# Linear attention, routed experts and an MLP on one core: array forms grouped, routing moved behind the masks, counts read in one load

## Chip, cores and metric

One core of a Trainium2 chip runs the whole program in one launch. The metric is the device time in microseconds (us) of that core; lower is better. Engines are TensorE (PE), VectorE (DVE), ScalarE (ACT), GpSimd (POOL) and SyncE (SP), each with its own instruction queue; they order one another by semaphores.

## What is computed

Three stages follow one another on 2 x 768 = 1536 tokens of width 384 (8 heads of 48):

```python
for t in range(S):                      # per batch and head, 48 x 48 state
    y[t] = r[t] @ (state + (u * k[t]) outer v[t])
    state = w[:, None] * state + k[t] outer v[t]
logits = x @ w_gate                     # 8 experts; x is y with its heads side by side
local = sigmoid(x @ w_local)
e[s] = argmax(logits[s]) if s == 0 or local[s] < 0.5 else e[s - 1]
out[s] = softmax(logits[s])[e] * relu(x[s] @ w1[e]) @ w2[e]
result = out + relu(layernorm(out) * g_ln @ w_ch1) @ w_ch2
```

## The kernel before

**Attention.** The 1536 tokens are 12 chunks of 128 (NT = 12), the two batches (B = 2) in turn. Inside a chunk the recurrence is a masked product. The loop of each engine runs over i from 0 to 13 and works on three chunks at once: the scores of chunk i, output and state of chunk j = i - 1, and the routing logits of chunk i - 2. PE's order in iteration i is written by hand: scores of chunk i (L1128, 8 products whose operands fill 64 rows and 128 columns of the array), the three transposes of chunk i - 2's rows X (L1135, 128 x 128), then the turned output of chunk j in bank 0: for each of 4 head pairs two products of the state (L1149, 64 rows x 48 columns) and two of the masked scores (L1152, 128 rows x 48 columns), which add to the same columns; then logits of chunk i - 2 (L1165, 128 x 128), addition to the state (L1176, 128 rows x 64 columns), and the four transposes that turn the output back (L1183, 128 x 128). Every fp32 product is two passes in the trace, every transpose one. So L1149 and L1152 show 16 passes each, in groups of four.

DVE in iteration i: stores X of chunk i - 2 (L836, adds the bonus term dv), masks the scores of chunk i (L846, two instructions), adds the state (stsum, L853), scales the next chunk's keys (kT, L825), then the bonus's diagonal (L863, L865). ACT copies the transposed X (L620) for the logits, the turned output (L629), the logits (L632), and multiplies v by the diagonal in 8 small instructions (L609), four before and four behind the copy L629. POOL multiplies rT, rk, ks and the state. SP starts the loads of a chunk: tin 512 KB, kr 384 KB, v 192 KB. ACT starts the first two experts' weights in halves of 1536 KB, in iterations 2, 4, 6 and 8 (HALF_WEIGHTS).

**Routing.** It comes in two phases: chunks 0 to 7 during iterations 10 to 12 and chunks 8 to 11 behind the loop. A phase is, on DVE, choose (argmax and codes, L762 to L771), carry_on (a scan over the tokens, L777 to L782), chosen (one-hot and gate value, L789 to L800) and places (row numbers, L808 to L819), with small products on PE between them. Then POOL scatters each chunk's rows to HBM, sorted by expert (L518, 8 and 4 indirect DMAs). SP fills the tail of an expert's rows with zeros and loads the first 256 rows (xrow, L433). Behind places of the second phase DVE computes counts and writes them to meta, of which each engine loads its registers one by one (expert_regs, L305).

**Experts.** Tiles of 256 rows, here eight, one for each expert. Each fp32 weight is split into two parts, high (split_hi, L359, ACT) and low (split_lo, L364, POOL and DVE), in six pieces of 1024 columns; pieces 0 to 2 are w1, 3 to 5 w2. A product is three passes (L1203, L1204, L1205). Expert 0's pieces 0 and 1 are made low by POOL in iterations 10 and 11, pieces 2 to 5 by DVE in iterations 9, 11, 12 and 13 (LATE_LO). When all are done, SP loads expert 2's weights (two halves) over expert 0's raw ones. Then comes the MLP, in three groups of four chunks, and POOL scatters its rows to the output (L599).

## Time and profile before

| | before |
|---|---|
| median of 3 runs | 424.46 us (423.89 to 425.12) |
| the profiled execution's own time | 423.79 us |
| its span, first to last instruction | 422.2 us |
| PE busy | 384.4 us (91%) |
| DVE / ACT / POOL busy | 217.3 / 146.5 / 137.5 us |
| chain that ended last | PE 81%, DVE 7%, DMA 4%, POOL 3% |

The span is 1.6 us short of the time. Busy shares are means over stages that differ; the chain that ended last follows back, from the last instruction, what released each step. A row of the timeline gives start, length, engine, line, operation and, in brackets, how long the engine was idle before it and who ended that.

### The profile page before, as it was taken

How to read it: one execution, taken by the hardware profiler on the slowest of the kernel's cores; microseconds unless marked ns; L12 is line 12 of the kernel's file. 1: busy time of each engine (PE TensorE's matmuls, PEld its weight loads, DVE VectorE, ACT ScalarE, POOL GpSimd, SP SyncE). 2: the span in 40 equal slices, each digit the busy share in tenths (PEclk: the TensorE clock that was granted, in tenths of full speed). 3: DMA queues.
4: the chain of work that ended last, by engine and by line, in shares of the span. 5: the costliest groups of instructions: out<-in, count | busy, mean ns of one | idle time of the engine just before them, and what ended most of it. 6: DMA issues, size and time to landing. Idle time of an engine off the chain costs nothing.

```text
span 422.2 us, 7567 instructions
## 1 busy us (share of the span) xinstructions
PE 384.4 (91%) x2768; PEld 342.1 (81%) x2768; DVE 217.3 (51%) x412; ACT 146.5 (35%) x295; POOL 137.5 (33%) x134
## 2 busy tenths in 40 slices
PE   6799999872089999999999998999999999999993
PEld 6566766531079999999999998889998899988993
DVE  5776568856127466374664779585213552133110
ACT  0354566630035537255382553542002320022000
POOL 5986775745122605325053240400110001100010
PEclk9899999965579999999999999999999999999998
DMA  6999881019646957749556150600100001100001
GB/s 202 347 334 363 314 289 46 2 58 335 219 143 170 351 197 262 270 163 385 190 195 258 30 241 0 191 0 2 37 20 19 1 2 37 39 0 2 19 20 37
DMA packets 17018, 61.07 MB, mean 145 GB/s; under 512 B 2128, under 2 KB 9808, under 8 KB 14672
## 3 DMA queue, kind: packets, MB, share of 16 engines
q1 hardware_dynamic: 12240, 25.87, 18.1%
q10 hardware_dynamic: 2304, 26.74, 17.5%
q0 software_dynamic: 2432, 7.92, 4.9%
q8 instruction: 24, 0.39, 0.4%
q14 instruction: 18, 0.15, 0.1%
HBM read 49.42 MB, written 11.10 MB: 143 GB/s over the span
## 4 chain that ended last, share of the span: by engine, by line
PE 81%; DVE 7%; DMA 4%; POOL 3%; issue 3%; ACT 1%; SPq 0%; DVEq 0%; ACTq 0%; POOLq 0%
PE bank L1203 21%; PE bank L1205 21%; PE bank L1204 21%; PE bank L1152 3%; PE bank L1149 3%; POOL xsort L518 3%; PE bank L1128 2%; DMA tin<-in_rkT 2%; PE bank L1198 1%; PE bank L1165 1%; PE bank L1183 1%; PE bank L1135 1%; DMA xsort<-X,cpos 1%; PE bank L1176 1%; DVE split L364 1%
## 5 line engine op out<-in xcount | busy, mean ns | idle before, releaser
L359 ACT CAST split<-raw 128x1024 fp32r<-128x1024 f32 (+1 forms) x60 | 59.2, 1004 | 0.0
L1203 PE MATMUL bank<-xT,split 128*128 128x256 f32 x192 | 55.2, 287 | 2.1 <-DVE xT L910 2.1
L1205 PE MATMUL bank<-xT,split 128*128 128x256 f32 x192 | 55.0, 286 | 0.0
L1204 PE MATMUL bank<-xT,split 128*128 128x256 f32 x192 | 55.0, 286 | 0.0
L599 POOL DMA_INDIRECT out<-orow,cpos x12 | 11.6, 970 | 132.7 <-DVE orow L1039 132.7
L364 DVE TENSOR_TENSOR split<-raw,split 128x1024 fp32r<-128x1024 f32 (+1 forms) x40 | 51.1, 1292 | 1.9 <-ACT split L359 1.7
L1203 PE MATMUL bank<-split,h2T 128*128 128x384 f32 x144 | 48.7, 338 | 0.0
L1205 PE MATMUL bank<-split,h2T 128*128 128x384 f32 x144 | 48.2, 335 | 0.0
L1204 PE MATMUL bank<-split,h2T 128*128 128x384 f32 x144 | 48.2, 335 | 0.0
L364 POOL TENSOR_TENSOR split<-raw,split 128x1024 fp32r<-128x1024 f32 (+1 forms) x20 | 45.7, 2302 | 6.3 <-ACT split L359 6.2
L718 ACT ACTIVATE h2T<-bank 128x512 fp32r<-128x512 f32 x36 | 21.5, 598 | 72.9 <-PE bank L1205 71.7
L1051 DVE SCALAR_TENSOR_TENSOR h2T<-bank,h2T 128x512 fp32r<-128x512 f32 x36 | 24.9, 691 | 37.5 <-ACT h2T L718 37.4
L1203 PE MATMUL bank<-split,hT 128*128 128x384 f32 x128 | 43.7, 341 | 0.0
L1203 PE MATMUL bank<-split 128*128 128x512 f32 x108 | 42.1, 390 | 1.2 <-DVE split L942 1.2
L1205 PE MATMUL bank<-split,hT 128*128 128x384 f32 x128 | 42.8, 335 | 0.0
L1204 PE MATMUL bank<-split,hT 128*128 128x384 f32 x128 | 42.8, 334 | 0.0
L676 ACT ACTIVATE hT<-bank 128x512 fp32r<-128x512 f32 x32 | 19.1, 597 | 67.3 <-PE bank L1205 67.3
L1205 PE MATMUL bank<-split 128*128 128x512 f32 x108 | 42.1, 390 | 0.0
L1204 PE MATMUL bank<-split 128*128 128x512 f32 x108 | 42.1, 390 | 0.0
L958 DVE SCALAR_TENSOR_TENSOR hT<-bank,hT 128x512 fp32r<-128x512 f32 x32 | 22.0, 687 | 36.5 <-ACT hT L676 36.5
L1203 PEld LDWEIGHTS bank<-xT,split 128*128 128x128 f32 x192 | 37.6, 196 | 2.5 <-DVE xT L910 2.5
L1204 PEld LDWEIGHTS bank<-xT,split 128*128 128x128 f32 x192 | 37.6, 196 | 0.0
(161 smaller groups left out, 704.5 us busy)
## 6 DMA issues: line engine op xcount, KB each, us to landing
raw<-in_wexp ACTq DMA_DIRECT2D x14, 1536.0 KB, 8.3
tin<-in_rkT SPq DMA_DIRECT2D x12, 512.0 KB, 6.5
kr<-in_rows_kr SPq DMA_DIRECT2D x12, 384.0 KB, 5.7
raw<-in_wch ACTq DMA_DIRECT2D x2, 2304.0 KB, 9.4
xsort<-zeros SPq DMA_DIRECT2D x8, 388.0 KB, 5.7
X<-xsort SPq DMA_DIRECT2D x8, 388.0 KB, 5.8
ysort<-yrow POOLq DMA_DIRECT2D x8, 388.0 KB, 7.2
raw<-in_wexp SPq DMA_DIRECT2D x2, 1536.0 KB, 10.0
```

The source lines that it names most:

```text
L359: act.copy(hi, src).then_inc(s_hi, 1)
L364: eng.tensor_tensor(lo, src, hi.bitcast(F32), ALU.subtract).then_inc(s_lop if c < POOL_CK else s_lod, 1)
L518: pool.indirect_dma_start(out=xsort, out_offset=bass.IndirectOffsetOnAxis(ap=cpos[:, j:j + 1], axis=0), in_=X[:, j, :], in_offset=None).th ...
L676: act.activation(hT[:, 0, x * FU:(x + 1) * FU, :], bank[HB[x]][:].rearrange("p (f t) -> p f t", f=FU), ACT.Relu).then_inc(m_h, 1)
L718: act.activation(h2T[:, f, 0, :], bank[HB2[f % 3]][:], ACT.Relu).then_inc(f_ra, 1)
L958: dve.scalar_tensor_tensor(out=hT[:, 1, q, :].rearrange("p f t -> p (f t)"), in0=bank[HB[x]][:], scalar=0.0, in1=hT[:, 0, q, :].rearrange( ...
L1051: dve.scalar_tensor_tensor(out=h2T[:, f, 1, :], in0=bank[HB2[f % 3]][:], scalar=0.0, in1=h2T[:, f, 0, :].bitcast(F32), op0=ALU.max, op1=AL ...
L1149: pe.matmul(bank[0][halves[h], n * P:(n + 1) * P], state[b][h * HALF:(h + 1) * HALF, n, :], rT[j % 3][h * HALF:(h + 1) * HALF, n, :], star ...
L1152: last = pe.matmul(bank[0][halves[h], n * P:(n + 1) * P], vn[j % VRING][:, 2 * n + h, :], sc[b][:, h, n, :], start=False, stop=True)
L1203: pe.matmul(dst, stationary[0], moving[0], start=first, stop=False)
L1204: pe.matmul(dst, stationary[0], moving[1], start=False, stop=False)
L1205: return pe.matmul(dst, stationary[1], moving[0], start=False, stop=last)
```

## The change

The diff stands with one line of context; a line "..." leaves unchanged lines out. On PE, the eight products of L1149 come first, then the eight of L1152, then the addition to the state, the transposes of X, those of the output, and the logits last; the waits for v and for the masked scores move between the two groups. On ACT the eight bonus products come first and the copy of the transposed X behind that of the output. On DVE the next keys are scaled ahead of stsum, choose(0) comes behind the masks, places(0) ahead of them, and of expert 0's low parts only piece 2 is made in the loop; pieces 3 to 5 are made in the first expert tile. SP loads w1 of expert 2 as soon as expert 0's w1 is split, ACT its w2 in the first tile. meta is laid out so that one load reads ten counts, without checks of their bounds.

```diff
@@ -119,10 +119,10 @@
-M_TILES, M_BEFORE, M_ROWS, M_ENDS, M_GROUP = (i * E for i in range(5))
-M_BEHIND = M_GROUP + NG
-M_MORE = M_BEHIND + 1
-meta = sb("meta", [1, M_MORE + 1], I32)
+M_TILES, M_MORE, M_BEHIND, M_GROUP = 0, E, E + 1, E + 2
+M_ROWS, M_ENDS = 2 * E, 3 * E
+assert M_GROUP + NG <= M_ROWS
+meta = sb("meta", [1, M_ENDS + E], I32)
@@ -297,25 +297,29 @@
 HALF_WEIGHTS = (2, 4, 6, 8)
-LATE_LO = (NT - 3, NT - 1, NT, NT + 1)
 def need(eng, s, n):
...
+def load_many(eng, a, b, most):
+    return nc.values_load_multi_w_load_instructions(
+        meta[0:1, a:b], engines=(eng.engine,), min_val=0, max_val=most,
+        skip_runtime_bounds_check_because="counts of rows that there are, and of their tiles")[1]
+
 def expert_regs(eng, offsets=False):
...
     eng.wait_ge(s_meta, 1)
-    tiles = [eng.value_load(meta[0:1, M_TILES + e:M_TILES + e + 1], min_val=1, max_val=NT) for e in range(E)]
+    said = load_many(eng, M_TILES, M_BEHIND + 1, NT + E)
+    tiles = [nc.s_assert_within(said[e], 1, NT, skip_runtime_bounds_check_because="counts rounded up to tiles, "
+                                "at least one") for e in range(E)]
+    more = nc.s_assert_within(said[M_MORE], 0, NT, skip_runtime_bounds_check_because="one less than a number of tiles")
     before = [0]
...
         before.append(eng.snap(before[e] + tiles[e], min_val=0, max_val=NT + E))
-    rows = [eng.value_load(meta[0:1, M_ROWS + e:M_ROWS + e + 1], min_val=0, max_val=TOK)
-            for e in range(E)] if offsets else None
-    behind = eng.value_load(meta[0:1, M_BEHIND:M_BEHIND + 1], min_val=0, max_val=NT + E)
-    more = eng.value_load(meta[0:1, M_MORE:M_MORE + 1], min_val=0, max_val=NT)
-    return tiles, before, rows, behind, more
+    rows = load_many(eng, M_ROWS, M_ROWS + E, TOK) if offsets else None
+    return tiles, before, rows, said[M_BEHIND], more
@@ -362,6 +366,13 @@
     eng.tensor_tensor(lo, src, hi.bitcast(F32), ALU.subtract).then_inc(s_lop if c < POOL_CK else s_lod, 1)
+
+def first_w1_split(eng):
+    eng.wait_ge(s_lop, POOL_CK)
+    eng.wait_ge(s_lod, CK // 2 - POOL_CK)
+
+def first_w2_split(eng):
+    eng.wait_ge(s_lod, CK - POOL_CK)
@@ -414,8 +425,8 @@
             sp.dma_start(gcol[:], gain_in).then_inc(s_small, 16)
-    split_done(sp, 0)
-    load_weights(sp, 2)
+    first_w1_split(sp)
+    load_weights(sp, 2, (0,))
@@ -431,8 +442,6 @@
     sp.dma_start(xrow[:], xsort[0:MT, 0:D].rearrange("(h p) d -> p h d", p=P)).then_inc(m_first, 16)
-    sp.wait_ge(s_meta, 1)
-
     sp.sem_inc(m_in, 16)
@@ -443,18 +452,17 @@
+    tiles, before, _, _, _ = expert_regs(sp)
     for e in range(E):
-        tiles = sp.value_load(meta[0:1, M_TILES + e:M_TILES + e + 1], min_val=1, max_val=NT)
-        before = sp.value_load(meta[0:1, M_BEFORE + e:M_BEFORE + e + 1], min_val=0, max_val=NT + E)
-        with sp.Fori(0, tiles) as i:
-            load_rows(before + i, nc.s_assert_within(
+        with sp.Fori(0, tiles[e]) as i:
+            load_rows(before[e] + i, nc.s_assert_within(
                 i * MT + e * CAP, e * CAP, e * CAP + TOK,
...
             sp.wait_ge(s_fill, 16 * (e + 2))
-    groups = [sp.value_load(meta[0:1, M_GROUP + g:M_GROUP + g + 1], min_val=1, max_val=NT + E)
-              for g in range(NG)]
+    groups = [nc.s_assert_within(x, 1, NT + E, skip_runtime_bounds_check_because="a group's rows are of one expert at least")
+              for x in load_many(sp, M_GROUP, M_GROUP + NG, NT + E)]
     for g in range(NG):
@@ -603,9 +611,9 @@
 def _(act):
-    def dg_times_v(j, heads):
+    def dg_times_v(j):
         b = j % B
-        for h in heads:
+        for h in range(H):
             last = act.activation(dv[b][:, h, :], vn[j % VRING][:, h, :], ACT.Copy, scale=dg[b][:, h:h + 1])
@@ -615,23 +623,20 @@
             load_weights(act, half // 2, (half % 2,))
-        if i >= 2:
-            act.wait_ge(s_xt, i - 1)
-            act.copy(xTa[:], bank[7][:, 0:D]).then_inc(s_xc, 1)
         j = i - 1
...
             need(act, s_x, j - B + 1)
-            dg_times_v(j, range(H // 2))
+            dg_times_v(j).then_inc(s_dvp, 1)
             act.wait_ge(s_yp, j + 1)
...
         if i >= 2:
+            act.wait_ge(s_xt, i - 1)
+            act.copy(xTa[:], bank[7][:, 0:D]).then_inc(s_xc, 1)
             act.wait_ge(s_lp, i - 1)
             act.copy(LG[:, i - 2, :], bank[7][:, D:D + E + 1]).then_inc(s_lg, 1)
-        if 0 <= j < NT:
-            dg_times_v(j, range(H // 2, H)).then_inc(s_dvp, 1)
         if NT - CK <= i < NT:
@@ -685,6 +690,9 @@
                 relus(range(NU))
+                if starts and e == 0:
+                    first_w2_split(act)
+                    load_weights(act, 2, (1,))
@@ -835,9 +843,9 @@
                               bank[4][:].rearrange("p (h d) -> p h d", h=H)[:, :, 0:Dh], dv[j % B][:], ALU.add).then_inc(s_x, 1)
-        if i == ROUTED[0]:
-            dve.wait_ge(s_late, 1)
-            choose(0)
+        if i == ROUTED[0] + 2:
+            places(0)
+            split_lo(dve, 0, POOL_CK)
         if i < NT:
@@ -845,15 +853,16 @@
                                   causal[:].unsqueeze(1).broadcast_to([P, NP, P]), ALU.mult).then_inc(s_sc, 1)
-        if i == ROUTED[0] + 2:
-            places(0)
+        if i + 1 < NT:
+            scale_k(i + 1)
         if 0 <= j < NT - B:
...
                               ALU.add).then_inc(s_ss, 1)
-        if i + 1 < NT:
-            scale_k(i + 1)
+        if i == ROUTED[0]:
+            dve.wait_ge(s_late, 1)
+            choose(0)
         if i < NT:
@@ -867,9 +876,6 @@
             chosen(0)
-        if i in LATE_LO:
-            split_lo(dve, 0, POOL_CK + LATE_LO.index(i))
-    assert len(LATE_LO) == CK - POOL_CK
@@ -886,8 +892,7 @@
     dve.tensor_scalar(meta[:, M_MORE:M_MORE + 1], cnt[:, 4, E - 1:E], 1.0, None, ALU.subtract)
-    dve.tensor_copy(meta[:, M_ROWS:M_ROWS + E], cnt[:, 0, :])
-    link(dve.tensor_tensor(meta[:, M_BEFORE:M_BEFORE + E], cnt[:, 5, :], cnt[:, 4, :], ALU.subtract))
+    link(dve.tensor_copy(meta[:, M_ROWS:M_ROWS + E], cnt[:, 0, :]))
     for g in range(NG):
@@ -948,6 +953,8 @@
     xT_lo()
+    for c in range(CK // 2, CK):
+        split_lo(dve, 0, c)
     for e in range(E):
@@ -1128,43 +1135,23 @@
             last.then_inc(s_scp, 1)
-        if i >= 2:
-            pe.wait_ge(s_x, i - 1)
-            need(pe, s_lg, i - 2)
-            for q in range(KD):
-                last = pe.transpose(bank[7][:, q * P:(q + 1) * P], X[:, i - 2, q * P:(q + 1) * P], ident[:])
-            last.then_inc(s_xt, 1)
-        if i == ROUTED[0] + 2:
-            counts(0)
         j = i - 1
...
-            pe.wait_ge(s_v[j % VRING], 16 * (j // VRING + 1))
-            pe.wait_ge(s_sc, 2 * (j + 1))
             need(pe, s_st, j - B + 1)
...
                     pe.matmul(bank[0][halves[h], n * P:(n + 1) * P], state[b][h * HALF:(h + 1) * HALF, n, :],
-                              rT[j % 3][h * HALF:(h + 1) * HALF, n, :], start=True, stop=False)
+                              rT[j % 3][h * HALF:(h + 1) * HALF, n, :], start=(n == 0), stop=False)
+            pe.wait_ge(s_v[j % VRING], 16 * (j // VRING + 1))
+            pe.wait_ge(s_sc, 2 * (j + 1))
+            for n in range(NP):
                 for h in range(2):
                     last = pe.matmul(bank[0][halves[h], n * P:(n + 1) * P], vn[j % VRING][:, 2 * n + h, :], sc[b][:, h, n, :],
-                                     start=False, stop=True)
+                                     start=False, stop=(n == NP - 1))
             last.then_inc(s_yp, 1)
-        if i == ROUTED[0]:
-            pe.wait_ge(s_late, 1)
-            code_rows(0)
-        if i == ROUTED[0] + 1:
-            expert_columns(0)
-        if i >= 2:
-            pe.wait_ge(s_xc, i - 1)
-            if i == 2:
-                pe.wait_ge(s_small, 16 * 2)
-            for q in range(KD):
-                last = pe.matmul(bank[7][:, D:D + E + 1], xTa[:, q * P:(q + 1) * P], wg[:, q, :],
-                                 start=(q == 0), stop=(q == KD - 1))
-            last.then_inc(s_lp, 1)
         if 0 <= j < NT - B:
@@ -1176,12 +1163,33 @@
             last.then_inc(s_u, 1)
+        if i == ROUTED[0] + 2:
+            counts(0)
+        if i >= 2:
+            pe.wait_ge(s_x, i - 1)
+            need(pe, s_lg, i - 2)
+            for q in range(KD):
+                last = pe.transpose(bank[7][:, q * P:(q + 1) * P], X[:, i - 2, q * P:(q + 1) * P], ident[:])
+            last.then_inc(s_xt, 1)
+        if i == ROUTED[0]:
+            pe.wait_ge(s_late, 1)
+            code_rows(0)
+        if i == ROUTED[0] + 1:
+            expert_columns(0)
         if 0 <= j < NT:
...
             last.then_inc(s_bk, 1)
+        if i >= 2:
+            pe.wait_ge(s_xc, i - 1)
+            if i == 2:
+                pe.wait_ge(s_small, 16 * 2)
+            for q in range(KD):
+                last = pe.matmul(bank[7][:, D:D + E + 1], xTa[:, q * P:(q + 1) * P], wg[:, q, :],
+                                 start=(q == 0), stop=(q == KD - 1))
+            last.then_inc(s_lp, 1)
@@ -1248,6 +1256,8 @@
             pe.wait_ge(m_y, n + XR)
+            if e == 0:
+                first_w2_split(pe)
             second(n, 0, range(KF // 2))
@@ -1268,7 +1278,10 @@
-        split_done(pe, e)
+        if e == 0:
+            first_w1_split(pe)
+        else:
+            split_done(pe, e)
         if e < E - 1:
```

## Rows read from the trace of the kernel before

**Rows 1.** Stretches: length; PE, PEld, DVE, ACT, POOL busy; clock, DMA share, GB/s.
```profile
19.30:44.00 24.70, 24.70 (x305) 16.88 (x304) 16.91 (x28) 11.72 (x44) 19.60 (x35) 1.00 0.94 340
84.70:91.50 6.80, 5.68 (x37) 2.71 (x37) 3.77 (x10) 1.38 (x5) 2.33 (x2) 0.50 0.00 0
118.80:122.20 3.40, 3.40 (x16) 3.40 (x17) 0.00 (x0) 0.00 (x0) 0.00 (x0) 0.50 0.17 26
122.30:263.00 140.70, 140.06 (x999) 139.37 (x998) 86.66 (x128) 71.57 (x100) 47.94 (x30) 1.00 0.57 208
```

**Rows 2.** Chain that ended last, iteration 4 and an expert tile: start, length, what.
```profile
38.43 1.09 PE bank L1128 x16
...
40.00 0.35 PE bank L1149 x4
...
42.83 0.77 PE bank L1165 x6
43.60 0.60 PE bank L1176 x16
44.20 0.59 PE bank L1183 x4
...
146.77 0.66 PE bank L1198 x6
```

**Rows 3.** Timeline of all engines, iteration 4: start, length, engine, line, operation.
```profile
39.45 0.55 PE L1135 MATMUL bank<-ident,X 128*128 128x128 f32 x3
39.57 1.29 DVE L846 TENSOR_TENSOR sc<-bank,causal 128x512 f32<-128x512 f32 x2 [0.54 <-PE bank L1128]
...
40.04 0.48 ACT L620 COPY xTa<-bank 128x384 f32<-128x384 f32 x1 [1.69 <-PE bank L1135]
...
40.78 0.34 DVE L853 TENSOR_TENSOR stsum<-state,bank 128x192 f32<-128x192 f32 x1
...
41.04 0.69 DVE L825 TENSOR_TENSOR kT<-tin,wn 128x512 f32<-128x512 f32 x1
```

**Rows 4.** Timeline of DVE around the routing, iterations 10 to 13.
```profile
70.73 0.21 DVE L762 TENSOR_REDUCE mx<-LG 128x8 f32<-128x64 f32 x1
...
72.04 1.28 DVE L846 TENSOR_TENSOR sc<-bank,causal 128x512 f32<-128x512 f32 x2
...
81.89 0.17 DVE L789 COPY ec<-bank 128x8 f32<-128x8 f32 x1 [1.14 <-PE bank L1095]
...
84.08 1.22 DVE L364 TENSOR_TENSOR split<-raw,split 128x1024 fp32r<-128x1024 f32 x1
...
86.87 0.18 DVE L808 COPY tot<-region 128x8 f32<-128x8 f32 x1 [1.10 <-PE bank L1105]
...
93.58 0.56 DVE L836 TENSOR_TENSOR X<-bank,dv 128x384 f32<-128x384 f32 x1 [3.68 <-ACT dv L609]
```

**Rows 5.** Chain that ended last, from the scatter to the expert products.
```profile
88.87 2.08 POOL xsort L518
...
103.19 0.96 POOL xsort L518
...
106.98 5.12 DMA xsort<-X,cpos
...
112.17 2.88 DMA xrow<-xsort
...
118.72 0.58 PE bank L1203
```

**Rows 6.** DMA issues: queue, operation, count, KB each, median us from issue to landing.
```profile
raw<-in_wexp ACTq DMA_DIRECT2D x14, 1536.0 KB, 8.3
...
out<-orow,cpos POOLq DMA_INDIRECT x12, 2.6
```

**Rows 7.** Timeline of DVE in the first expert tile.
```profile
123.34 0.69 DVE L958 SCALAR_TENSOR_TENSOR hT<-bank,hT 128x512 fp32r<-128x512 f32 x1 [4.68 <-ACT hT L676]
```

**Rows 8.** Timeline of PE, iteration 12.
```profile
85.82 0.90 PE L1135 MATMUL bank<-ident,X 128*128 128x128 f32 x3 [2.71 <-DVE X L836]
```


## The prediction

> **What bounds the kernel now.** I read the busy time by stretch first. PE has no idle time in the attention loop (24.70 of 24.70 us, clock 1.00, which is 2.4 GHz), and none to speak of once the expert products run (140.06 of 140.70 us) [rows 1]. What lies between is the routing. So only two things can shorten this kernel: less PE time in the loop's iterations, and an earlier first expert product, at 118.72 us [rows 5]. What follows that product isn't touched and should come through unchanged, 303.5 us of the 422.2 us span.
>
> The chain through iteration 4 shows what an iteration is made of: 1.09 for the scores, 0.48 for the transposes of X (40.00 - 38.43 - 1.09), eight groups of four passes at 0.35 to 0.36 (together 42.83 - 40.00 = 2.83), 0.77 logits, 0.60 state, 0.59 transposes back: 6.36 us [rows 2]. Six transposes that run between products of the same form take 0.66 us, 0.11 each; three of them cost 0.48 and four 0.59 where the form changes before and behind them, so a change costs 0.14 to 0.15 us [rows 2]. A group of four passes is two pairs (the two heads of a pair run together) at 0.107 each, and 0.14 for the change: 0.355.
>
> **The change, part by part.**
>
> *Grouping the products.* L1149 and L1152 alternate eight times, which is eight changes; grouped there are two. Six go: 6 x 0.14 = 0.84 us per iteration. Each group becomes 8 x 0.107 + 0.14 + 0.01 = 1.01 us. Behind L1152 comes L1176, also 128 rows by half the columns, so that change may go too (0.14), and the two kinds of transposes and the logits are all 128 x 128: two more at 0.15. PE alone would need 6.36 - 0.84 - 0.44 = 5.1 us. It can't have it, for two waits that the old order covered.
>
> First wait, at L1176. It needs stsum of the same iteration, and stsum now stands behind kT. The scores start at 39.45 - 1.09 = 38.36; the masks start 1.21 later [rows 3]. Masks 1.21 (39.57 to 40.78), kT 0.69 less the 0.08 by which a follower overlaps it, stsum 0.34, hand-over 0.05: DVE is ready at 1.21 + 1.21 + 0.61 + 0.34 + 0.05 = 3.42 us. PE is there at 1.09 + 1.01 + 1.01 - 0.14 = 2.97 to 3.05. It waits some 0.4 us.
>
> Second wait, at the logits. Transposes of X start at 3.42 + 0.60 = 4.02. From their start to the end of ACT's copy took 40.04 + 0.48 - 39.45 = 1.07, and 0.05 to hand over [rows 3]: 5.14 us. Transposes back are done by 4.85, so PE waits 0.3 us. The logits take 0.77 [rows 2], and the iteration ends at 5.91 us.
>
> So an iteration shrinks by 0.45 us, not by 1.28. Iteration 1 has no such waits yet, and I take 0.7 there; iterations 2 to 9 are eight: 0.7 + 8 x 0.45 = 4.3 us at the start of iteration 10, which was at 38.36 + 5 x 6.36 = 70.16.
>
> *Bonus first on ACT.* ACT is busy 11.72 us in 24.70, which is 3.0 us of each 6.36 [rows 1]; of those, its copy of X alone is 0.48 [rows 3], so the eight products are at most 2.5. They now come in one piece at the start of an iteration, from iteration 6 on behind a high part of the weights (1 us). That ends at 3.5 at the latest; the turned output is made at 3.1, and its copy is wanted only by 4.35, behind the transposes of X. I cost it at nothing; if the copy came later still, each tenth would be a tenth in the six iterations from 6 on.
>
> *Routing of the first phase.* From iteration 10 on DVE sets the pace. Its work in sequence: masks at 1.21; from there to the end of the diagonal of iteration 11 it had 81.89 - 1.14 - 72.04 = 8.71 us without a wait; choose takes 72.04 - 70.73 = 1.31 and now lies inside; chosen 84.08 - 81.89 = 2.19; storing X 0.48; places and the hand-over 88.87 - 86.87 = 2.00 [rows 4, 5]. Sum: 15.9 us from the start of iteration 10 to the first scatter, against 18.7 before. What went are the split at 84.08 (1.14) and the waits of 1.14 and 1.10 us; choose, which lay beside PE's scores, gives 0.6 back.
>
> *Second phase and scatter.* Behind places comes one split (1.14), then X of chunk 11 at 16.8. From there to the second phase's scatter it took 103.19 - 93.58 = 9.61 us [rows 4, 5], and that work is the same: 26.4. But POOL needs 2.38 + 7 x 1.26 = 11.2 us for the eight indirect DMAs of the first phase (1.26 from the three steps between 103.19 and 106.98), so it is free at 27.1: POOL, not DVE, is late next. The last of four is issued at 27.1 + 3.8 = 30.9. It took 5.12 to land [rows 5], while the zeros moved, and both halves of expert 2's weights had started only behind DVE's last split (93.58 + 0.48 + 1.14, about 95.2); the output's scatters land in 2.6 [rows 6]. Now half of those weights start about 10 us before it, and the other half much later. Between the two I take the middle, 3.9: 34.8. From landing to the first expert product it is 118.72 - 112.10 = 6.62 [rows 5]: 41.4 us, against 118.72 - 70.16 = 48.6. That is 7.1 us.
>
> *Counts in one load.* No register load is on the chain; what released PE was xrow, landed at 112.17 + 2.88 [rows 5]. The counts are made behind places of the second phase, which moves forward by 4.3 + (103.19 - 70.16) - 26.4 = 10.9 us, and xrow by 4.3 + 7.1 = 11.4. The old loads would have lost half a microsecond of their cover, and cost at most that. One load costs nothing, and I book no gain. On SP and POOL the fewer loads lie beside PE's first tile.
>
> *Three low parts in the first tile.* DVE waits 4.68 us there before its first relu part [rows 7]; three splits at 1.14 take 3.4. Free. ACT starts expert 2's w2 behind its last relu of the tile, and reads it behind the first relu of the next. Between them PE has the 48 passes of w2 and 18 of w1, at the mean of 140.70 / 999 = 0.14 us [rows 1] 9.3 us; such a load lands in 8.3 [rows 6]. Free, with a microsecond to spare; beyond it ACT's high parts for expert 2 would be late, which PE reads a tile later. SP's start of w1, now before the zeros, is a queue entry more in front of them and one fewer behind.
>
> *Clock.* PE idles through the second phase and begins the expert products at 0.50 of its clock, for the 3.4 us of one row; the other cold row lasted 6.8 [rows 1]. Half clock costs at most half of its time, so a start as long as the other would cost 3.4 x 0.5 = 1.7 us more, and one as short nothing. It is nearest to the row at its own place; I take 0.3.
>
> **Sum.** 4.3 + 7.1 - 0.3 = 11.1 us. The profiled execution took 423.79 us (span 422.2 and 1.6 around it); it becomes 412.7. The median of the runs is 0.7 above that execution: 413.4 us.
>
> **Rivals.**
>
> *Grouping brings nothing (0.12).* If the 0.14 us belonged to each head pair and not to the change of form, both groups take 4 x 0.355 = 1.42 us. L1176 then starts at 3.93 with no wait for stsum, and the logits at 3.93 + 0.60 + 1.12 = 5.65; the iteration lasts 6.42. The loop loses 0.5 instead of winning 4.3, the routing keeps its 7.1: 423.8 - 6.3, or 418.2 us as a median. Against it: no gap stands between transposes and products of one form [rows 2]. The Trainium skill would land there too by another way (TensorEngine Tiling, Gotcha 1: PSUM Pressure): different row tiles cannot use one PSUM bank at the same time, and the two heads of L1149 lie in different rows and write bank 0. By that a grouped L1149 would take its 16 passes in turn, 1.7 us or more. The trace disagrees: four such passes and the change fit into 0.35 us, where four in turn at 0.107 would be 0.43 alone.
>
> *Neither wait holds (0.10).* If DVE and ACT keep up, PE's 5.1 us isn't reached either, since two iterations move 2 x 1088 + 1536 KB = 3.8 MB, at 340 GB/s [rows 1] 11.2 us: 5.6 each. Then 8 x 0.3 = 2.5 us more are won: 410.9.
>
> *The scatter's landing stays (0.12).* Eight scatters, the zeros and expert 2's w1 still share the engines. With 5.1 us or a bit more instead of 3.9, and most of the clock's 1.7: 415.8.
>
> *Slower (0.04).* The clock. It fell to 0.50 (1.2 GHz) in the stretch from 84.7 [rows 1], and before that PE had waited 2.71 us in one piece; transposes then took 0.90 instead of 0.55 [rows 3, 8]. If the new waits of 0.4 and 0.3 us in every iteration did the same, PE's 5.1 us would be 1.7 times as long, 8.7, with the waits near 9.4: 8 x 3.0 = 24 us lost against 7 won, 441 us. It decides only if the waits grow from 0.7 us in two pieces to something like that 2.71, so I think little of it.
>
> **Numbers.** The forecast has 0.60, and 0.02 is left for no difference. The likeliest time is 413.4. The range runs from 409.5 (neither wait, landing in 2.6) to 418.5 (grouping brings nothing). Faster has the first four cases, 0.94; same within 0.3% 0.02, slower 0.04; 0.3% is about what a measurement of this kernel can tell from no change.
>
> **What would show it.** L1149 and L1152 as two groups of 16 passes at about 1.0 us each; iterations of 5.9 us; DVE's stsum as releaser of L1176 and ACT's copy as releaser of L1165; first scatter near 81.7 and no gap of 3 us before the ninth; last landing near 100.6; first expert product near 107.5; everything behind it 303.5 us long. I am wrong if iterations stay at 6.3 or more, if PE's clock falls in the loop, or if the stretch behind the first expert product grows.

## The result, and the profile after

| | before | after | forecast for after |
|---|---|---|---|
| median of 4 runs | 424.17 us (423.07 to 425.12) | 419.82 us (419.32 to 420.19) | 413.4 |
| the profiled execution | 423.79 us, span 422.2 | 420.02 us, span 417.7 | 412.7 |
| start of iteration 10 | 70.15 | 66.88 | 65.9 |
| first scatter | 88.87 | 88.43 | 81.7 |
| last scatter landed | 112.10 | 106.38 | 100.6 |
| first expert product | 118.72 | 113.08 | 107.5 |
| from there to the end | 303.45 | 304.60 | 303.5 |

The ratio is 0.9876 (95% interval 0.9839 to 0.9912): faster by 1.2%, 4.4 us where 11 were forecast, and outside the range of 409.5 to 418.5. The forecast went wrong at the first scatter. It stands where it stood, although the loop in front of it is 3.3 us shorter.

The page of the changed kernel, busy time of each engine:

```profile
PE 375.7 (90%) x2768; PEld 349.0 (84%) x2768; DVE 216.6 (52%) x411; ACT 146.5 (35%) x295; POOL 132.9 (32%) x134
```

PE lost 8.7 us of busy time and the kernel 4.4 us of time.

**The loop.** The timeline of PE in iteration 4 of the changed kernel (start, length, engine, line, operation, in brackets the idle time before it and who ended that):

```profile
30.94 1.16 PE L1135 MATMUL bank<-rT,kT 64*128 64x128 f32 x16
32.03 1.08 PE L1146 MATMUL bank<-rT,state 64*48 64x128 f32 x16
33.04 1.08 PE L1152 MATMUL bank<-sc,vn 128*48 128x128 f32 x16
34.45 0.67 PE L1163 MATMUL bank<-vn,ks 128*64 128x48 f32 x16 [0.33 <-DVE stsum L861]
35.05 0.55 PE L1172 MATMUL bank<-ident,X 128*128 128x128 f32 x3
35.43 0.60 PE L1183 MATMUL bank<-ident,yTs 128*128 128x128 f32 x4
36.17 0.84 PE L1190 MATMUL bank<-wg,xTa 128*128 128x9 f32 x6
36.93 1.16 PE L1135 MATMUL bank<-rT,kT 64*128 64x128 f32 x16
```

Two groups of 16 passes at 33.04 - 32.03 = 1.01 us each, then the wait for stsum, as forecast. It ends at 34.45 - 30.94 = 3.51 us after the scores began, and the step had put it at 3.42; the iteration lasts 36.93 - 30.94 = 5.99 us (forecast 5.91; before 6.36 [rows 2]). One iteration, the third, takes 6.54. There POOL, behind the constants of the routing, makes rT while DVE makes kT. The timelines of DVE and of POOL:

```profile
25.61 1.29 DVE L854 TENSOR_TENSOR sc<-bank,causal 128x512 f32<-128x512 f32 x2 [1.51 <-PE bank L1135]
26.82 1.23 DVE L833 TENSOR_TENSOR kT<-tin,wn 128x512 f32<-128x512 f32 x1
27.97 0.34 DVE L861 TENSOR_TENSOR stsum<-state,bank 128x192 f32<-128x192 f32 x1
```

```profile
26.22 1.28 POOL L533 TENSOR_TENSOR rT<-tin,wp 128x512 f32<-128x512 f32 x1
27.45 1.47 POOL L552 TENSOR_TENSOR ks<-kr,wnT 128x384 f32<-128x384 f32 x1
```

kT takes 1.23 us instead of 0.69 [rows 3]: the first 0.68 lie beside rT, which ends at 27.50. The masks and stsum, which have one input in PSUM, keep their length beside POOL's work (1.29 for the two masks, 0.34 for stsum, as in [rows 3]).

**The first routing.** Timelines of the changed kernel from 69.9 us, first DVE, then POOL, then PE:

```profile
69.90 0.34 DVE L861 TENSOR_TENSOR stsum<-state,bank 128x192 f32<-128x192 f32 x1
70.16 0.21 DVE L770 TENSOR_REDUCE mx<-LG 128x8 f32<-128x64 f32 x1
70.41 0.59 DVE L772 TENSOR_TENSOR le<-LG,mx 128x64 f32<-128x64 f32 x1
71.03 2.27 DVE L773 TENSOR_TENSOR sel<-le,code 128x64 f32<-128x64 f32 x1
73.33 0.22 DVE L774 TENSOR_REDUCE ac<-sel 128x8 f32<-128x64 f32 x1
73.46 0.72 DVE L776 SCALAR_TENSOR_TENSOR fr<-LG,first 128x8 f32<-128x8 f32 x1
74.22 0.17 DVE L778 TENSOR_TENSOR gc<-fr,ac 128x8 bf16<-128x8 f32 x1
```

```profile
70.32 0.59 POOL L560 TENSOR_TENSOR state<-stsum,wst 128x192 f32<-128x192 f32 x1 [2.96 <-DVE stsum L861]
70.87 2.34 POOL L368 TENSOR_TENSOR split<-raw,split 128x1024 fp32r<-128x1024 f32 x1
73.17 0.99 POOL L543 TENSOR_TENSOR rk<-kr 128x384 f32<-128x384 f32 x1
```

```profile
70.99 0.55 PE L1172 MATMUL bank<-ident,X 128*128 128x128 f32 x3
74.53 0.46 PE L1093 MATMUL bank<-identb,gc 128*2 128x128 bf16 x4 [3.00 <-DVE gc L778]
```

Read DVE against POOL. The multiplication at L773, 64 elements a partition, takes 2.27 us and ends at 73.30; POOL's low part ends at 73.21. L776, with 8 elements, takes 0.72 us and ends at 74.18; POOL's rk ends at 74.16. L774 between them, a reduction with one input, takes its 0.22. So the operations with two inputs in SBUF end when POOL's instruction ends. The choice, with the second le that follows these rows, takes 4.28 us to the start of the next instruction at 74.44 (4.2 in the texts of the experiments), where the same seven instructions took 1.31 before (72.04 - 70.73 [rows 4]). The Trainium skill has this as a rule (SBUF — State Buffer, Who interferes with whom): a DVE instruction with two inputs in SBUF contends with a GpSimd instruction that reads SBUF, since both use a shared port pair, and that pair is an exclusive lock. The rows agree: L773 waits for all that is left of POOL's 2.34 us.

PE stands 3.00 us for the codes, with the transposes back, the logits and the next scores queued behind them. Its clock falls to 0.50 (1.2 GHz) at 74.7, just behind the wait; the windows (busy time of PE, PEld, DVE, ACT, POOL, then the granted clock, DMA share and GB/s) of the changed kernel show the loop, that wait, what follows it, and the start of the experts:

```profile
18.40:44.00 25.60, 23.22 (x325) 19.72 (x324) 16.57 (x29) 12.92 (x47) 20.58 (x37) 1.00 0.94 336
70.30:74.40 4.10, 1.15 (x19) 0.89 (x19) 3.96 (x7) 0.87 (x2) 3.84 (x3) 1.00 0.00 0
74.70:81.50 6.80, 6.80 (x52) 5.96 (x51) 5.63 (x11) 3.07 (x11) 0.70 (x1) 0.50 0.01 2
113.10:119.00 5.90, 5.90 (x27) 5.90 (x28) 4.02 (x4) 1.53 (x2) 0.82 (x1) 0.50 0.43 135
```

PE is busy all 6.80 us at 0.50, where the scores take 2.01 us instead of 1.09. Iteration 10 lasts 77.05 - 66.88 = 10.17 us. Now DVE, late itself, has to wait for PE as well, three times before the first scatter. These are the three rows of its timeline:

```profile
79.17 1.29 DVE L854 TENSOR_TENSOR sc<-bank,causal 128x512 f32<-128x512 f32 x2 [1.00 <-PE bank L1135]
...
82.98 0.17 DVE L797 COPY ec<-bank 128x8 f32<-128x8 f32 x1 [1.20 <-PE bank L1102]
...
86.42 0.17 DVE L816 COPY tot<-region 128x8 f32<-128x8 f32 x1 [0.76 <-PE bank L1112]
```

From the start of iteration 10 to the first scatter it is 88.43 - 66.88 = 21.55 us; the forecast had 15.9, and before it was 18.7.

**Scatter and landing.** The chain of waits of the changed kernel behind the first scatter:

```profile
99.67 0.96 POOL xsort L526
...
103.47 2.91 DMA xsort<-X,cpos
106.44 2.97 DMA xrow<-xsort
109.46 1.56 PE bank L1206 x6
```

The gap of 3 us ahead of the ninth scatter is gone, all twelve run at POOL's pace (88.43 to 103.47 is 15.04 us, forecast 15.0), and the last lands in 2.91 us instead of 5.12 [rows 5].

### The profile page after: what moved, and what is told of

Its sections match the earlier page's. It is cut to its first block, busy times and chain, and to the rows that moved or that the text cites. A ratio compares the mean times of both kernels' runs of the same rounds, so it can differ in the third digit from the quotient of the medians.

```text
span 417.7 us, 7375 instructions
## 1 busy us (share of the span) xinstructions
PE 375.7 (90%) x2768; PEld 349.0 (84%) x2768; DVE 216.6 (52%) x411; ACT 146.5 (35%) x295; POOL 132.9 (32%) x134
## 4 chain that ended last, share of the span: by engine, by line
PE 77%; DVE 9%; issue 4%; POOL 3%; DMA 3%; ACT 2%; SPq 1%; DVEq 0%; POOLq 0%; ACTq 0%
PE bank L1211 22%; PE bank L1213 22%; PE bank L1212 22%; PE bank L1135 3%; POOL xsort L526 3%; PE bank L1190 2%; DMA tin<-in_rkT 2%; DVE sc L854 2%; PE bank L1206 1%; DVE kT L833 1%; PE bank L1163 1%; PE bank L1146 1%; PE bank L1172 1%; ACT xTa L637 1%; PE bank L1152 1%
## 5 line engine op out<-in xcount | busy, mean ns | idle before, releaser
L368 DVE TENSOR_TENSOR split<-raw,split 128x1024 fp32r<-128x1024 f32 (+1 forms) x40 | 49.5, 1255 | 2.1 <-ACT split L363 1.9
L1211 PEld LDWEIGHTS bank<-xT,split 128*128 128x128 f32 x192 | 38.1, 199 | 2.5 <-DVE xT L915 2.5
L1212 PEld LDWEIGHTS bank<-xT,split 128*128 128x128 f32 x192 | 38.1, 198 | 0.0
```

The source lines that it names most:

```text
L368: eng.tensor_tensor(lo, src, hi.bitcast(F32), ALU.subtract).then_inc(s_lop if c < POOL_CK else s_lod, 1)
L1211: pe.matmul(dst, stationary[0], moving[0], start=first, stop=False)
L1212: pe.matmul(dst, stationary[0], moving[1], start=False, stop=False)
```

## The experiments

Ten kernels, each in three rounds against the kernel before on the same chip; the ratios compare across chips, the medians only roughly (the kernel before had a median of 424.2 to 426.3 us beside them). "Routing" is from the scores of iteration 10 to the first scatter; times are of the profiled execution.

| kernel | median us | ratio, 95% interval | iteration | routing | first expert product | rest |
|---|---|---|---|---|---|---|
| before | 424.17 | 1 | 6.36 | 18.7 | 118.72 | 303.45 |
| changed | 419.82 | 0.9876 (0.9839 to 0.9912) | 5.99 | 21.55 | 113.08 | 304.60 |
| choice ahead of the masks | 414.17 | 0.9741 (0.9689 to 0.9793) | 5.99 | 16.50 | 107.95 | 303.52 |
| stsum first | 414.08 | 0.9750 (0.9696 to 0.9804) | 5.44 | 21.32 | 107.46 | 303.74 |
| both | 409.82 | 0.9627 (0.9597 to 0.9658) | 5.44 | 16.31 | 102.71 | 304.31 |
| both, POOL's part earlier | 409.05 | 0.9578 (0.9550 to 0.9606) | 5.44 | 15.52 | 103.27 | 303.60 |
| POOL's parts later | 417.87 | 0.9819 (0.9761 to 0.9877) | 5.99 | 19.75 | 112.50 | 304.29 |
| no POOL parts | 413.85 | 0.9739 (0.9682 to 0.9797) | 5.99 | 16.54 | 107.87 | 303.48 |
| codes late | 417.58 | 0.9828 (0.9765 to 0.9892) | 5.99 | 19.63 | 111.74 | 303.78 |
| grouping alone | 417.61 | 0.9818 (0.9768 to 0.9869) | 5.54 | 19.52 | 112.63 | 303.56 |
| single loads | 419.79 | 0.9840 (0.9821 to 0.9858) | 5.99 | 21.61 | 114.29 | 304.67 |
| low parts in the loop | 422.54 | 0.9900 (0.9873 to 0.9927) | 5.99 | 21.96 | 116.57 | 304.60 |

### The place of the choice

```diff
+                if i == ROUTED[0]:
+                    dve.wait_ge(s_late, 1)
+                    choose(0)
                 if i < NT:
                     b = i % B
                     dve.wait_ge(s_scp, i + 1)
...
-                if i == ROUTED[0]:
-                    dve.wait_ge(s_late, 1)
-                    choose(0)
```

> The changed kernel with choose(0) put back ahead of the masks of iteration 10, nothing else. Changed: 419.8 us, choose(0) 4.1 us long there (70.16 to 74.22), of which 2.27 is one 128x64 multiply beside a POOL split; PE waits 3.00 us for its codes, then the clock is at 0.50 for 6.8 us. Theory A (the multiply is held up by POOL's split, which is what makes PE wait and the clock fall): choose runs while POOL is idle, takes 1.2 to 1.4 us, PE waits under 0.5 us at the code products, the clock holds 1.00 until about 84, the first scatter is at 82.5 to 84 instead of 88.4, time 413.5 to 416. Rival B (the new iteration's waits bring the clock down by themselves): clock still falls near 75, first scatter no earlier than 86, time 418 or more.

Measured: 414.17 us, as theory A expected, and within a microsecond of the forecast of the whole. The timeline of DVE and of PE in this kernel:

```profile
67.74 0.23 DVE L772 TENSOR_TENSOR le<-LG,mx 128x64 f32<-128x64 f32 x1
68.00 0.22 DVE L773 TENSOR_TENSOR sel<-le,code 128x64 f32<-128x64 f32 x1
...
68.40 0.16 DVE L776 SCALAR_TENSOR_TENSOR fr<-LG,first 128x8 f32<-128x8 f32 x1
...
77.91 2.15 DVE L798 TENSOR_TENSOR oh<-ec,code 128x64 bf16<-128x64 f32 x1
```

```profile
71.70 0.55 PE L1172 MATMUL bank<-ident,X 128*128 128x128 f32 x3
72.18 0.38 PE L1093 MATMUL bank<-identb,gc 128*2 128x128 bf16 x4
```

The same instructions are back at 0.16 to 0.23 us, PE finds the codes ready, and its clock stays at 1.00 until 84.1. The first scatter stands at 16.5 us. One of these operations is still held: oh, 2.15 us, beside POOL's second low part (77.63 to 79.98).

### Is it POOL that holds DVE?

First, POOL's two low parts moved from iterations 10 and 11 to 11 and 12:

```diff
-                if NT - B <= i < NT:
-                    split_lo(pool, 0, i - NT + B)
+                if NT - B + 1 <= i < NT + 1:
+                    split_lo(pool, 0, i - NT + B - 1)
```

> The changed kernel with POOL's two low parts of expert 0 one iteration later (11 and 12 instead of 10 and 11), choose(0) where the change puts it, behind the masks. Theory A (contention): with no split beside it choose(0) takes 1.3 to 2.2 us (POOL's rk may still hold one operation up for up to 1 us), PE waits 0.2 to 1.3 us, the clock holds, time 414 to 416.5. Rival C (the place behind masks, keys and stsum is what makes PE wait, contention is a detail): PE still waits 2 us or more, the clock falls, time 418.5 to 420.

The choice fell from 4.28 to 2.37 us and PE's wait from 3.00 to 1.09 us, and the clock held, but the time came out at 417.87, above the 414 to 416.5 expected. The timeline of DVE in iteration 11 of this kernel says why:

```profile
80.45 2.16 DVE L798 TENSOR_TENSOR oh<-ec,code 128x64 bf16<-128x64 f32 x1
...
82.66 2.25 DVE L802 TENSOR_TENSOR sel<-ec,code 128x64 f32<-128x64 f32 x1
```

POOL's two parts ran back to back from 80.17 to 84.83, and held two later operations of the same chain, 2.0 us each. The contention was moved, not removed. (In the profiled execution the whole loop also stands 1.5 us later, which this edit can't have caused; see the last section.) Second, and later, the parts were taken away from POOL, with the orders of DVE and PE untouched. This kernel leaves the low part of the first two pieces of expert 0's weights out, so its output is not right and it stands for its times alone:

```diff
             act.copy(hi, src).then_inc(s_hi, 1)
+            if job == 0 and c < POOL_CK:
+                act.copy(lo, src).then_inc(s_lop, 1)
...
-                if NT - B <= i < NT:
-                    split_lo(pool, 0, i - NT + B)
```

> The changed kernel without GpSimd's two low parts in iterations 10 and 11; ScalarE copies the raw weights into their place behind its high parts (1 us each), so the first two eighths of the first expert's weights have a wrong low part. Nothing of VectorE's or TensorE's order is touched. Theory (two-operand work of VectorE in SBUF waits for GpSimd's instruction): the second product of the choice takes under 1 us instead of 2.27, held by GpSimd's rk of iteration 11 at most, which now follows the state at once; the choice takes 1.3 to 2.3 us instead of 4.2, TensorE waits under 1.3 us for it instead of 3.00 and keeps its clock; the comparison of L798 takes 0.2 us instead of 2.15 in iteration 11. First scatter 16 to 17.3 us behind the scores of iteration 10 instead of 21.55, and time 413.8 to 415.3 (ratio 0.976 to 0.979). Rival (the choice is slow at its new place for another reason, such as its own chain of hand-overs): it keeps its 4.2 us, the first scatter its 21.5, and the time stays at 419.8 (0.9876).

With the choice at its new place, the timelines of DVE and PE in this kernel:

```profile
70.36 0.59 DVE L772 TENSOR_TENSOR le<-LG,mx 128x64 f32<-128x64 f32 x1
70.99 0.92 DVE L773 TENSOR_TENSOR sel<-le,code 128x64 f32<-128x64 f32 x1
...
72.08 0.15 DVE L776 SCALAR_TENSOR_TENSOR fr<-LG,first 128x8 f32<-128x8 f32 x1
...
78.84 0.23 DVE L798 TENSOR_TENSOR oh<-ec,code 128x64 bf16<-128x64 f32 x1
```

```profile
72.58 0.38 PE L1093 MATMUL bank<-identb,gc 128*2 128x128 bf16 x4 [1.09 <-DVE gc L778]
```

413.85 us and 16.54 us of routing: the rival (slow for another reason) is out. The 0.92 that is left ends with POOL's rk, which runs from 70.83 to 71.83 here. That the routing is as long as with the choice ahead of the masks (16.50) is a coincidence. Without POOL's parts oh is free too, 0.23 us where the other kernel pays 2.15, and up to ec, the copy just ahead of oh (L797), the new place still takes 78.65 - 66.84 = 11.81 us, against 77.72 - 67.11 = 10.61 at the old one. Most of these 1.2 us are le and sel beside POOL's state and rk (0.59 and 0.92, against 0.23 and 0.22).

### DVE's delay, or PE's stop and its clock?

The changed kernel with PE's code products of the first phase behind the scores of iteration 11:

```diff
                     last.then_inc(s_scp, 1)
+                if i == ROUTED[0] + 1:
+                    pe.wait_ge(s_late, 1)
+                    code_rows(0)
...
-                if i == ROUTED[0]:
-                    pe.wait_ge(s_late, 1)
-                    code_rows(0)
```

> The changed kernel, with TensorE's code products of the first phase moved from iteration 10 (between X's transposes and the transposes back) behind the scores of iteration 11. The choice itself stays where the change put it, beside GpSimd's low part, and lasts its 4.2 us. It parts two things that came together in the changed kernel: VectorE's 2.9 us of delay, and the 3.00 us that TensorE stood still behind it, with the clock at 0.50 for 6.8 us after. Theory (both cost): TensorE passes on to the transposes back, the logits and the scores of iteration 11, waits under 1 us for the codes, and the clock stays at 1.00 until VectorE falls behind for good, near 84. The delay of VectorE alone is left: 16.5 us (choice ahead of the masks) + 2.9 = 19.4 us from the scores of iteration 10 to the first scatter, instead of 21.55: 2.1 us less, time 417.7 (ratio 0.985). Rival 1 (only VectorE's delay counts, the clock was without effect because VectorE set the pace anyway): the first scatter stays at 21.5 us, time 419.8 (0.9876). Rival 2 (only TensorE's stop counts): 16.5 us, 414.5 (0.976).

Routing took 19.63 us, time 417.58, as the theory expected; the clock held from 34.0 until 81.7, 2 us less than expected. (A stretch of half clock from 30.5 to 34.0, in iteration 4, lies far ahead of the edit and makes that iteration, and with it the first expert product, a microsecond longer.) DVE and PE in this kernel's timeline:

```profile
71.69 2.27 DVE L773 TENSOR_TENSOR sel<-le,code 128x64 f32<-128x64 f32 x1
```

```profile
75.21 0.38 PE L1093 MATMUL bank<-identb,gc 128*2 128x128 bf16 x4 [0.53 <-DVE gc L778]
```

Both count. Of the 21.55 - 16.50 = 5.05 us that the new place of the choice costs, 21.55 - 19.63 = 1.9 us are PE's stop with the half clock behind it, and 3.1 us DVE's delay. The 1.9 is what is left of a larger loss. At ec (L797) the changed kernel stands at 82.98 - 66.88 = 16.10 us, this one at 81.28 - 67.54 = 13.74, so 2.4 us are lost there already, and the wait at L816 comes on top. But its oh then comes late enough to be held for a short time only, 0.86 us instead of 2.15 here, and that gives 1.3 back. No run parts PE's stop from the half clock.

### The order in the loop

The changed kernel with stsum ahead of kT again:

```diff
-                if i + 1 < NT:
-                    scale_k(i + 1)
                 if 0 <= j < NT - B:
                     dve.wait_ge(s_u, j + 1)
...
                                       ALU.add).then_inc(s_ss, 1)
+                if i + 1 < NT:
+                    scale_k(i + 1)
```

> The changed kernel with stsum ahead of the scaling of the next keys again on DVE. Predicted from the first trace: PE's wait for stsum (0.33 us per iteration) goes, the iteration falls from 5.99 to 5.6 us, 8 x 0.38 = 3.0 us off at iteration 10: 416.8. Rival: something else is late at once (the masked scores, the copy for the logits) and takes over half or more of it: 418.3 or more. choose(0) still stands beside POOL's split, so the routing keeps its 21.5 us from iteration 10 to the first scatter.

And the kernel before with nothing but the grouping:

```diff
-                                      rT[j % 3][h * HALF:(h + 1) * HALF, n, :], start=True, stop=False)
+                                      rT[j % 3][h * HALF:(h + 1) * HALF, n, :], start=(n == 0), stop=False)
+                    for n in range(NP):
                         for h in range(2):
...
-                                             start=False, stop=True)
+                                             start=False, stop=(n == NP - 1))
```

> The kernel before with one edit: in each iteration L1149's eight products first, then L1152's eight; all orders and places otherwise as before (424.2 us). If a change of the array's form costs 0.14 us and nothing new is waited for, an iteration falls from 6.36 to 5.52 us, or to about 5.6 if the loads bound it: 7 us off by iteration 10, 417 to 418 us. If new waits of 0.3 to 0.4 us appear here too, 5.9 us and 420 to 421.

Windows of the kernel with stsum first, and of the one with the grouping alone, in the loop:

```profile
19.00:44.00 25.00, 24.47 (x369) 21.63 (x366) 19.93 (x34) 14.94 (x53) 22.35 (x38) 1.00 0.98 361
```

```profile
19.00:44.00 25.00, 25.00 (x347) 20.75 (x345) 19.22 (x32) 13.60 (x51) 21.53 (x36) 1.00 0.94 359
```

Grouping alone came out as expected, at 417.61 us. It gives 6.36 - 5.54 = 0.82 us an iteration, six changes of form at 0.14. All that the change did to the loop's order beyond it made the loop slower, 5.99. With stsum first the iteration is 5.44, no wait for stsum stands in the loop, and the third iteration takes 5.44 as well. So kT ahead of stsum costs 0.55 us an iteration, and the rest of the new order wins 0.10. The time, 414.08, was 2.7 us better than the 416.8 expected: 2.0 us of it because iterations fell to 5.44 and not 5.6, the third one too, and 0.9 because the half clock at the start of the experts was shorter (rest 303.74 instead of 304.60). The DMA engines then move 361 GB/s and are busy 98% of the time, so the 340 of [rows 1] was what the kernel before asked for, and no ceiling. The grouping alone (0.9818) stands at or ahead of the whole change (0.9876); the intervals overlap, so the rest of the change, as it stands, has won nothing that can be measured.

### The other parts

Both of DVE's orders put back:

> The changed kernel with both orders on DVE put back: choose(0) ahead of the masks, stsum ahead of the next keys. If the two losses are separate (5.0 us in iterations 2 to 9, 5.6 in the routing with its clock), the gains add: 419.8 - 5.7 - 5.7 = 408.4; iterations of 5.44 us, first scatter 16.5 us behind the start of iteration 10, PE's wait for the codes under 0.3 us. If they overlap (the clock falls anyway, or the scatters and loads are late next), 411 to 413.

409.82 us (408.4 expected if they add), ratio 0.9627: the two gains add, 0.0135 and 0.0126 in the ratio alone and 0.0249 together. Then POOL's second low part ahead of its state in iteration 11, so that it is over before oh:

```diff
+                if i == NT - 1:
+                    split_lo(pool, 0, 1)
                 j = i - 2
                 if 0 <= j < NT - B:
```

> As e5_both, and POOL makes its second low part of expert 0 ahead of the state of iteration 11 instead of behind it, so that it no longer runs beside the one-hot of the routing (2.15 us there instead of 0.92). If contention is what makes the one-hot long, it falls to 0.9 to 1.3 us and the first scatter comes 0.9 to 1.3 us earlier than in e5_both: 407.3 to 407.8. If the part hits another operation instead (the rku product or the state that PE's last chunk needs), no gain, within 0.4 us of e5_both.

The timeline of DVE in iteration 11 of this kernel:

```profile
72.81 1.36 DVE L874 TENSOR_TENSOR rku<-rk,ub 128x384 f32<-128x384 f32 x1
...
74.86 0.23 DVE L800 TENSOR_TENSOR oh<-ec,code 128x64 bf16<-128x64 f32 x1
```

oh is free at 0.23, rku is held instead (1.36 against 0.55), and 16.31 - 15.52 = 0.8 us of the 1.9 are won in the routing. The time, 409.05, is above the 407.3 to 407.8 expected. It is the lowest here, but its interval (to 0.9606) still overlaps that of the kernel with both orders put back (from 0.9597), so that this step makes the whole kernel faster is likely, but not shown.

The counts again in single loads:

```diff
-            return nc.values_load_multi_w_load_instructions(
...
+            return [eng.value_load(meta[0:1, q:q + 1], min_val=0, max_val=most) for q in range(a, b)]
```

> The changed kernel, with the ten counts read by one load each, without the checks of bounds (the changed kernel: one load, 419.8 us). Predicted as forecast: nothing, within 0.4 us, since xrow lands 6 us behind the counts and only then does PE go on. Rival: the loads reach past the landing, 1 us or more, 420.8 or later.

0.984 (0.9821 to 0.9858) beside 0.9876 (0.9839 to 0.9912): no cost that can be measured, as forecast. From PE's first transpose of xrow to the first expert product it is 114.29 - 110.67 = 3.62 us, and 113.08 - 109.46 = 3.62 in the changed kernel.

Low parts 2 to 5 back in iterations 9 and 11 to 13, and both halves of expert 2's weights started by SP behind them, as in the kernel before:

```diff
...
+                if i in LATE_LO:
+                    split_lo(dve, 0, POOL_CK + LATE_LO.index(i))
...
-            first_w1_split(sp)
-            load_weights(sp, 2, (0,))
+            split_done(sp, 0)
+            load_weights(sp, 2)
...
```

> The changed kernel with expert 0's low parts back in iterations 9, 11, 12 and 13 on DVE, and expert 2's weights loaded by SP in one go behind them; all else as changed (419.8 us). By the forecast the split before X of chunk 10 delays the first scatter by 1.1 us, and the last scatter, with 3 MB of weights beside it, lands in 4.7 to 5.1 us instead of 2.9: first expert product 3 us later, 422.5 to 423.2. Rival: the split is hidden behind PE's waits and the landing doesn't depend on the load: 420.5 or less.

The chain of waits of this kernel at the landing:

```profile
104.41 5.54 DMA xsort<-X,cpos
```

422.54 us, as expected. The last scatter lands in 5.54 us instead of 2.91, and 21.96 - 21.55 = 0.4 us are lost ahead of the first scatter, where 1.1 was expected. That makes 3.0 us for the part of the change that moves low parts and halves the load, nearly all of it in the landing. The ratios agree where they share a chip: 0.9900 against 0.9840 for the single loads, which cost nothing, is 2.6 us. The weight load was started 104.41 - 91.96 = 12.4 us ahead of the last scatter here and 103.47 - 89.53 = 13.9 us ahead of it in the changed kernel, so that its size, 3 MB instead of 1.5, is the likelier cause of the long landing; no run parts the two.

## Why the prediction was wrong

**The step that failed** is *Routing of the first phase*: "choose takes 72.04 - 70.73 = 1.31 and now lies inside", in the sum of 15.9 us. It carried the duration of DVE's instructions to another place without asking what POOL does there. Between stsum and the diagonal POOL is released by stsum to its state, its low part and rk, and the choice waits for them: 4.28 us instead of 1.31, which is 2.97. The same step said that from iteration 10 on DVE sets the pace, and gave PE's stop for the codes no term. PE stood 3.00 us, its clock fell to 0.50, and DVE then waited 1.00 + 1.20 + 0.76 = 2.96 us for PE. The other terms of the sum came out 0.3 us shorter (rku took 0.55 us instead of 0.95). The whole was measured at 21.55 us; with the choice at its old place it was 16.50, and without POOL's parts 16.54. This one step is 5.65 of the 7.3 us by which the profiled execution missed.

The trace of the kernel before showed the effect, in rows that I had summed over. These are two rows of its timeline, of DVE and of POOL, inside the stretch of 8.71 us and the chosen step:

```profile
82.09 0.92 DVE L790 TENSOR_TENSOR oh<-ec,code 128x64 bf16<-128x64 f32 x1
```

```profile
80.57 2.35 POOL L364 TENSOR_TENSOR split<-raw,split 128x1024 fp32r<-128x1024 f32 x1
```

An operation of 0.23 us took 0.92 and was over with POOL's (80.57 + 2.35 = 82.92). I read the length of the step (2.19) and not its rows.

The rest of the account, of the profiled execution (forecast 412.7, measured 420.02):

| step | forecast | measured | missed by |
|---|---|---|---|
| start of iteration 10 | 65.86 | 66.88 | +1.0 |
| from there to the first scatter | 15.9 | 21.55 | +5.65 |
| first to last scatter | 15.0 | 15.04 | 0 |
| landing | 3.9 | 2.91 | -1.0 |
| landing to first expert product | 6.62 | 6.70 | +0.1 |
| from there to the end (303.5 and 0.3 of clock) | 303.8 | 304.60 | +0.8 |
| time outside the span | 1.6 | 2.3 | +0.7 |

*Grouping.* Right in mechanism and price (1.01 us a group, 0.14 a change of form); the wait for stsum was where the text put it. Missed by 0.08 in each iteration, since the wait for stsum ended 0.09 later than worked out, and by 0.55 more in the third, whose long kT is the same contention again. What the text did not ask is what the new order was good for: it costs 0.55 us an iteration.

*Bonus first on ACT* was costed at nothing. PE waits for ACT's copy 0.14 us an iteration (0.7 in five), where 0.3 was forecast, and no run took this part alone.

*Second phase and scatter.* POOL was late next, as the text said. The landing was taken halfway between 5.12 and 2.6, which was a guess, and came to 2.91; the run with the old low parts and the old load gave 5.54, so it is these two together that make it long, the size of the load more likely than its time.

*Counts, and low parts in the first tile.* Nothing, as forecast, so far as the runs can tell: the part behind the first expert product is 303.5 us in the kernels with a short half clock, whether these low parts lie in the first tile or not (303.52 and 303.45).

*Clock.* The text allowed 1.7 us for a longer cold start of the experts and took 0.3. The half clock lasted 6.0 us there (113.08 to 119.1) instead of 3.5, which is worth half of 2.5 us, and the rest is 1.15 us longer.

*Rivals.* That grouping brings nothing, and that the landing stays, are out. That neither wait holds did not happen in the changed kernel; with stsum first one of them goes, and the floor of 5.6 us an iteration that I put under that case was passed (5.44). The slower case had the right mechanism at the wrong place: it asked for a wait of about 2.71 us in one piece, looked for it in the loop, and it came once, 3.00 us, in the routing, at a price of 1.9 us together with the half clock. Its reading of [rows 8] was loose as well: the clock of the kernel before fell at 84.7, inside the wait that ended at 85.82, when PE had stood 1.6 us and not 2.71.

What stays open: whether ACT's order costs anything by itself, whether it is the size or the time of the weight load that makes the landing long, and why the time outside the span varies, 1.6 to 2.6 us over these kernels.

## What to carry to other kernels

A duration from a trace belongs to its place: before moving a DVE operation, read what POOL runs beside the new place, and check every two-input operation against the end of POOL's. An order that looks like a gift to one engine (kT early, the choice behind the masks) has to be priced against the engine that waits in program order behind it. And a small operation that holds up PE can cost more than its own length: here the 3 us of waiting were followed by 6.8 us at half clock, and the two together cost 1.9 us beyond DVE's own delay.

## What the runs showed of the hardware

A two-input DVE operation of 8 or 64 elements a partition takes 0.16 to 0.23 us alone and up to 2.27 us beside a 2.35 us instruction of POOL. Reductions (L774, 0.22, beside rk) and operations with an input in PSUM (the two masks 1.29, stsum 0.34) kept theirs. It goes the other way too: ks took 1.47 us instead of 1.0 behind kT in the third iteration.

The half clock at the start of the expert products lasts 3.5 to 6.1 us, and the rest of the kernel is longer by about half of what is over 3.5: 303.48 us behind 3.5 us of it, 303.56 and 303.74 behind 3.9, 304.31 behind 5.4, 304.60 behind 6.0. At the start of the kernel it lasts 3.4 us in some profiled executions and 6.8 in others (of the best version among them), and then the whole loop stands 1.1 to 1.6 us later; the single loads and POOL's later parts differ from the changed kernel only behind iteration 9 and show it too, so it isn't their edit.
